# Attention, gated MLP and routed experts on one core: conditional steps nested in each other, the last waits and the first group rearranged

## The reference

```python
scores = scale * np.matmul(q, k.transpose(0, 1, 3, 2))
mask_local = (rel >= 0) & (rel < 32)                        # heads 0 to 3
mask_strided = (rel >= 0) & (pos[None, :] % 32 == pos[:, None] % 32)   # heads 4 to 7
attn = softmax(np.where(masks[None, :, :, :], scores, -1000000000.0))
x = np.matmul(attn, v)                                      # (B, S, H * 64) = 2304 x 512
...
xn = x / rms * rms_g
g = xn @ w_gate                                             # 512 x 1536
x = silu(g) * (xn @ w_val) @ w_out                          # 2304 x 512
...
logits = x @ w_gate + modality_bias[modality_id]            # 8 experts
e_idx = np.argmax(logits, axis=1)
for e in range(E):
    mask = e_idx == e
    h = np.maximum(x[mask] @ w1[e], 0.0)                    # 512 x 1024
    out[mask] = gate_w[mask, None] * (h @ w2[e])
```

## Time and profile before

| | us |
|---|---|
| three runs | 920.97, 921.89, 925.51 |
| median | 921.89 |
| the profiled execution | 922.88 |
| its span | 921.00 |
| mean granted clock of TensorE | 0.991 of full |

### The profile page before, as it was taken

The page is one execution under the profiler, slowest core; times in us unless marked ns, Lnnn a source line. Parts: engine busy times, 40 slices in busy tenths (PEclk is TensorE's granted clock), DMA queues, the critical chain, the costliest instruction groups (busy, mean ns, idle before and its releaser), DMA issues.

```text
span 921.0 us, 15739 instructions
## 1 busy us (share of the span) xinstructions
PE 888.2 (96%) x5388; PEld 758.4 (82%) x5397; DVE 464.4 (50%) x1253; ACT 368.7 (40%) x944; POOL 307.3 (33%) x367
## 2 busy tenths in 40 slices
PE   8989999999999999999999999999999999999993
PEld 5657899888878888889999999898787888888882
DVE  5864554433454435533432242873876446666651
ACT  5866512534354444521121122143354335545530
POOL 2744772244323433244234333151132222211220
PEclk9998999999999999999999999999999999999997
DMA  8983122222204110211121111536245735555520
GB/s 180 258 193 95 39 64 61 70 74 62 61 24 128 50 35 24 69 36 35 36 80 35 46 50 54 190 97 240 92 162 183 270 137 191 195 207 192 188 70 24
DMA packets 76075, 98.94 MB, mean 107 GB/s; under 512 B 38813, under 2 KB 42909, under 8 KB 76000
## 3 DMA queue, kind: packets, MB, share of 16 engines
q1 hardware_dynamic: 72320, 86.70, 31.0%
q0 software_dynamic: 3680, 11.28, 3.6%
HBM read 88.52 MB, written 10.22 MB: 107 GB/s over the span
## 4 chain that ended last, share of the span: by engine, by line
PE 84%; DVE 8%; issue 3%; ACT 2%; DMA 1%; POOL 1%; DVEq 0%; SPq 0%; ACTq 0%; POOLq 0%
PE ps L1143 33%; PE ps L1182 14%; PE ps L1644 10%; PE ps L1629 10%; PE ps L1075 3%; PE ps L1104 2%; PE ps L1085 2%; PE ps L1656 2%; PE ps L1052 2%; PE ps L1209 1%; PE ps L1202 1%; DMA w_raw<-in_moe_w 1%; PE ps L585 1%; DVE w_lo L1863 1%; PE ps L1725 1%
## 5 line engine op out<-in xcount | busy, mean ns | idle before, releaser
L1461 DVE SCALAR_TENSOR_TENSOR h<-h,ps 128x384 f32<-128x384 f32 x72 | 39.9, 554 | 176.5 <-ACT h L1319 176.5
L949 POOL TENSOR_TENSOR sm<-sm,rinv 72x288 f32<-72x288 f32 (+1 forms) x51 | 45.6, 894 | 208.0 <-DVE rinv L1405 207.9
L1143 PE MATMUL ps<-x_hi,gate_hi 128*128 128x384 f32 x288 | 104.7, 363 | 0.1
L1143 PE MATMUL ps<-x_hi,val_hi 128*128 128x384 f32 x288 | 101.8, 353 | 0.5 <-DVE h L1467 0.5
L1143 PE MATMUL ps<-x_hi,gate_lo 128*128 128x384 f32 x288 | 97.7, 339 | 0.0
L979 POOL CAST out_hi<-out_raw 128x512 fp32r<-128x512 f32 x72 | 45.8, 637 | 154.3 <-DMA out_raw<-in_moe_w_out 154.3
L981 POOL TENSOR_TENSOR out_lo<-out_raw,out_hi 128x512 fp32r<-128x512 f32 x72 | 95.3, 1324 | 5.8
L1143 PE MATMUL ps<-x_hi,val_lo 128*128 128x384 f32 x288 | 96.6, 335 | 0.0
L1143 PE MATMUL ps<-x_lo,val_hi 128*128 128x384 f32 x288 | 96.5, 335 | 0.0
L1143 PE MATMUL ps<-x_lo,gate_hi 128*128 128x384 f32 x288 | 94.8, 339 | 0.0
L1182 PE MATMUL ps<-out_hi,h_hi 128*128 128x512 f32 x216 | 89.4, 414 | 2.1 <-DVE h_lo L1472 2.1
(11 more groups left out here) (270 smaller groups left out, 1919.1 us busy)
## 6 DMA issues: line engine op xcount, KB each, us to landing
w_raw<-in_moe_w SPq DMA_DIRECT2D x72, 512.0 KB, 6.4
out_raw<-in_moe_w_out SPq DMA_DIRECT2D x72, 256.0 KB, 2.7
x_rows<-y_tiles SPq DMA_DIRECT2D x18, 256.0 KB, 2.7
early_w_raw<-in_moe_w SPq DMA_DIRECT2D x8, 512.0 KB, 6.6
gate_raw<-in_moe_w_gate SPq DMA_DIRECT2D x4, 768.0 KB, 10.2
val_raw<-in_moe_w_val SPq DMA_DIRECT2D x4, 768.0 KB, 10.4
qk<-in_q SPq DMA_DIRECT2D x8, 288.0 KB
qk<-in_k SPq DMA_DIRECT2D x8, 288.0 KB
```

The lines of the kernel that those rows point to most:

```text
L949: pool.tensor_tensor(s3, s3, rinv[0:n, i, :].unsqueeze(2).to_broadcast([n, 4, c]), ALU.mult).then_inc(s_no, 1)
L1143: mm = pe.matmul(ps[:, bank, 0:CH], w[:, i, kk, cols], x[:, kk, :], start=(m == 0), stop=(m == n - 1))
L1461: dve.scalar_tensor_tensor(out=hf[n % 2][:, :], in0=hf[n % 2][:, :], scalar=1.0, in1=ps[:, 0, 0:CH], op0=ALU.add, op1=ALU.mult).then_inc(s ...
```

## The change

In the tables, group 19's exponentials, inversion and normalisation each move back by one tick. In DVE's tick 19, x_lo moves behind `mask_max(19)`. The start of PE has ten fillers ahead of the first scores where it had six, and they stand at other places. The conditional steps go through a new function, `while_live`, which puts each further step inside the `If` of the one ahead of it; the load of `final` moves ahead of them. POOL's conditional waits go through the same function, and `s_last` is waited for behind them.

```diff
-EXPS = {j: SCORE[j] + (0 if j < HEAD else 1) for j in range(G)}
-INVERT = {j: SCORE[j] + (1 if j < HEAD else 3) for j in range(G)}
-NORM = {j: SCORE[j] + (1 if j < HEAD else 4) for j in range(G)}
+
+EXPS = {j: SCORE[j] + (0 if j < HEAD - 1 else 1) for j in range(G)}
+INVERT = {j: SCORE[j] + (1 if j < HEAD - 1 else 2 if j < HEAD else 3) for j in range(G)}
+NORM = {j: SCORE[j] + (1 if j < HEAD - 1 else 2 if j < HEAD else 4) for j in range(G)}
...
+        def while_live(eng, n_used, do, t=None):
+
+            t = SURE if t is None else t
+            if t < STEPS:
+                with eng.If(n_used > t - 1):
+                    do(t)
+                    while_live(eng, n_used, do, t + 1)
+
...
-            for t in range(SURE, STEPS):
-                with eng.If(n_used > t - 1):
-                    step(t, t % 4)
-            last(eng.value_load(final[0:1, 0:1], min_val=NTT - 1, max_val=SLOTS - 1))
+            s = eng.value_load(final[0:1, 0:1], min_val=NTT - 1, max_val=SLOTS - 1)
+            while_live(eng, n_used, lambda t: step(t, t % 4))
+            last(s)
...
-                pe.wait_ge(s_mr, 1)
...
+            keep_busy(7)
+            pe.wait_ge(s_mr, 1)
             pe.wait_ge(s_cst, 2)
             pe.wait_ge(s_zero, 4)
-            keep_busy(6)
             for s in range(TICKS):
                 if s < EARLY:
                     for key in QK_AT.get(s, []):
+                        if s == 0 and key[2] == 2:
+                            keep_busy(1)
                         turn_qk(*key)
+                if s == 0:
+                    keep_busy(2)
...
                     normalise_x(x)
-                    if x == 0:
-                        x_split(x)
...
                     mask_max(j)
+                if s == SPREAD[0] + 1:
+                    x_split(0)
...
+
+            def arrived(t):
+                if live(t, -AHEAD):
+                    pool.wait_ge(s_xg[(t + AHEAD) % 4], 16 * ((t + AHEAD) // 4 + 1))
+                pool.wait_ge(s_out[t % 2], 16 * ((t - 2) // 2 + 1))
+
+            while_live(pool, n_used, arrived)
             pool.wait_ge(s_last, 16)
-
-            for t in range(SURE, STEPS):
-                with pool.If(n_used > t - 1):
-                    if live(t, -AHEAD):
-                        pool.wait_ge(s_xg[(t + AHEAD) % 4], 16 * ((t + AHEAD) // 4 + 1))
-                    pool.wait_ge(s_out[t % 2], 16 * ((t - 2) // 2 + 1))
```

## The result

The changed kernel takes **915.15 us** (median of 7 runs, 912.5 to 916.59), the one before 921.89 (7 runs beside them, 919.83 to 942.47). The ratio is 0.9919, 95% interval 0.9894 to 0.9945, so 5 to 10 us faster. The profiled execution has a span of 913.2 us against 921.0, 7.8 less; the medians differ by 6.7.

The account below looks back on a forecast made before the run. TensorE, busy 96% of the span, was taken as the bound. Gains of 2.1 + 1.8 + 1.85 + 1.2 = 6.95 us gave 915.9 by the profiled execution, 914.9 by the median, so 915.4; range 911.8 to 918.8.

Parts of the forecast that it names:

- Last steps nested: Conditional steps at the end: one failed test leaves all, hT_lo starts earlier; 2.1 us gained, 1.1 to 2.6 possible.
- So I keep one stall of 1.8 us: DVE at the end: one test and one 1.8 us stall remain, so hT_lo starts at 899.8 instead of 901.89.
- tie with DVE: Kernel before, tail: PE's sequencer has the last slot's number only at 902.9, level with DVE.
- POOL's last waits: POOL's end: twelve branches run while the last scatter flies, so the closing drain starts and ends earlier; 1.8 us gained.
- the rival of the tied drain: POOL's end: the drain ends with what the scatter began, so no gain there; 917.2 us, chance 0.20.
- Exps and x_lo: Near 60 us: moving group 19's exponentials and x_lo closes PE's 1.95 us idle time; 1.85 us gained, bounds 0 and 1.95.
- 0.1 is late next: Near 60 us: PE's next score wants qT at 61.7, ACT evacuates it up to 61.8, so 0.1 us is lost.
- the gap moves to the next waiter: Near 60 us: the gap moves in full to qT on ACT or x_lo; 917.3 us, chance 0.05.
- Start: First scores on PE: rearranged fillers raise the clock earlier; 1.2 us or more gained, or 0.3 lost if it does not rise.
- Clock rises no sooner: Start of PE: the fillers bring no earlier clock rise, 1.5 us more; 916.9 us, chance 0.15.
- Clock stays up at more places: From 70 to 78 us and at the last product the clock no longer falls; first stretch 3.4 us, 912.0, chance 0.12.
- slower: Between 60 and 84 us the clock falls more often; 931 us with four low stretches, chance 0.03 shared with another rival.

Follow-up runs that it names:

- e10: The changed kernel with the last tile's 24 products reordered, the 16 reading hT_hi first, then the 8 reading hT_lo; 914.41 us.
- e2: The kernel before with only POOL's last waits nested and put ahead of the wait for the last scatter; 920.87 against 921.25 us, ratio 0.9993.
- e12: The changed kernel with x_lo back ahead of the mask on DVE, group 19's exponentials still a tick later; 915.21 against 920.35 us, ratio 0.9932.

## Why the prediction came out, point by point

**Last steps nested: 2.1 forecast, 1.04 in the trace, just under the lower bound of 1.1.** The step that failed is "So I keep one stall of 1.8 us". The 1.79 of the earlier trace rows is what is left of the stall behind the fifth flat test. It was counted as the whole price of a far jump, and the tests ahead of it as a cost beside it. The two overlap: one test and its jump take 2.8 to 3.1 us. So hT_lo came 2.2 us behind the transposes, not 1.2. That PE has one far test left, hidden, was right, though it lasts 3.4 to 3.7 us and not 2.8. The second mistake was to carry the 1.34 us from hT_lo to PE's first matmul over as one number. It came out as 1.41, but only because two changes cancel. It is not a wait for hT_lo; it is the load of a flag and a report, as e10 showed. In the kernel before the report came 1.05 us behind hT_lo and PE's product 0.28 behind that, held up by PE's own sequencer, so the "tie with DVE" was none. In the changed kernel the flag's load took 0.60 us instead of 0.32, the report came 1.33 behind hT_lo, and PE followed in 0.07. The longer load is no chance: with the steps nested and the load of `final` ahead it takes 0.50 to 0.61 us in every profile, in the six others 0.32. Why stays open.

**POOL's last waits: 1.8 forecast, 1.76 here, 1.75 in e2.** Right by its mechanism; the rival of the tied drain is out.

**Exps and x_lo: 1.85 forecast, 1.07 in the first profile.** The gap closed as written. What failed is the step "0.1 is late next": the prediction looked at ACT's qT and not at the transposes of q and k ahead of it, whose load of k landed inside the 1.95 us in the kernel before. The rival "the gap moves to the next waiter" is half true, with another waiter. Over the profiles the next gap is 0 to 1.12 us, so the term is worth 0.8 to 1.95, and 1.7 more where the clock would have fallen behind the gap. The move of x_lo is worth 0.9 of it where the load of k is early (e12).

**Start: 1.2 forecast, 1.88 in the profile.** The mechanism was right, the clock is up at the first scores, and 1.4 us lie between the first two as written. The term was too small in two places. The chain to the first scores is 0.30 us shorter (9.34 to 9.04) where it was to be 0.27 longer, since the clock was up at 7.35 and the second eight transposes took 0.86 us instead of 1.19; and the stretch up to the third scores gave 0.44 where 0.28 was counted. Nor is the size a property of one profile. It depends on when the clock would have risen without the fillers, 6.4 to 18.5 us; against a rise at 18.5 it is 4.4 us by the first gate product. The Trainium skill ("TensorE: Matmul & The Clock Gate", Part 1) has the throttle released by activity, and seven of seven filled starts agree, while the same unfilled work had it released anywhere between 6.4 and 18.5 us.

**The rivals of the clock.** "Clock rises no sooner" is out. "Clock stays up at more places" came true between 70 and 78 (1.38 us) and was paid back at 597.9 (1.56 us); ahead of the last products' end the clock fell for 3.4 us as before. No further low clock in sum, so "slower" had nothing to stand on.

So 915.4 met 915.15 in part by luck: two terms that were too large (by 1.1 and 0.8) were made up for by one too small (by 0.7) and by a wait for weights in the profile of before (2.25) that the change does not touch. By the profiles alone the forecast was 915.9 and the measurement is 914.94.

## What to carry to other kernels

- The idle time left behind a row of tests is not the price of a jump: count from the first test, and look at every engine that takes the same jump, since the one with the larger code can be the later one.
- Ahead of a wait for several semaphores ask which comes last, not which is named in the code beside it; here a report that "nothing is to be done" came last, and dropping it, with the products put in an order that hides hT_lo, gave 4.35 us in the trace (2.76 of idle time, the rest clock) where trimming the jump had given 1.
- When a gap closes, look one instruction further on PE for a load that used to land inside it. And judge a change of the clock by the spread of the times, not by one profile.

## What the runs showed of the hardware that was not expected

- The conditional jump over the steps that don't run costs 2.8 to 3.1 us on DVE, from the test to the next instruction, and on PE the test that takes such a jump lasts 2.7 to 3.7 us.
- The same start gave a full clock at 6.4 us or only at 18.5 us, in executions of kernels with the same first 50 us.
- An idle time of 1.95 us on PE was followed, 0.9 to 2.0 us behind its end, by 3.4 us of half clock in four of six profiles, in all three with an early rise; one of 1.3 us at 65 to 76 us in eleven of fourteen; and the 3.5 to 5.5 us ahead of the last product by 3.4 or 6.8 us of it in all thirteen. With 0.81 us in that place it was not.
- POOL's drain at the end is 3838 ns in every one of fourteen traces, whatever stands ahead of it.
